# A recurrent block and two mixers on one core: early jobs placed anew, y of four chunks kept, table loaded first

## What is computed

```
cur      = (u * k_t) outer v_t
y_t      = r_t @ (state + cur)
state    = w_t[:, None] * state + k_t outer v_t
```

```
h   = gelu(x @ w_in)            # 384 -> 1024, tanh form
u,v = halves of h
v_n = (v - mean) / sqrt(var + 1e-6) * g_ln
v_s = w_sg @ v_n + b_sg         # over the 768 steps
x   = x + (u * v_s) @ w_out
```

## Time and profile before

| | us | share of the span |
|---|---|---|
| median of three runs | 441.37 | |
| the profiled execution | 443.14 | |
| its span, first to last instruction | 441.6 | |
| PE busy | 411.4 | 93% |
| DVE busy | 203.4 | 46% |
| POOL busy | 165.4 | 37% |
| ACT busy | 110.7 | 25% |
| mean granted clock of PE | 0.961 of full | |

### The profile page before, as it was taken

The page is one execution under the profiler, slowest core; times in us unless marked ns, Lnnn a source line. Parts: engine busy times, 40 slices in busy tenths (PEclk is TensorE's granted clock), DMA queues, the critical chain, the costliest instruction groups (busy, mean ns, idle before and its releaser), DMA issues.

```text
span 441.6 us, 6914 instructions
## 1 busy us (share of the span) xinstructions
PE 411.4 (93%) x2682; PEld 395.5 (90%) x2682; DVE 203.4 (46%) x414; ACT 110.7 (25%) x218; POOL 165.4 (37%) x174
## 2 busy tenths in 40 slices
PE   6869798878598999999999999999999999999997
PEld 5759788767497999998999999999999999999996
DVE  5747946766475595623165465635013113212311
ACT  3445222343524111205730021234013003201300
POOL 6746444635514484434769999200000000000000
PEclk9988958998888999999999999999999999999999
DMA  9997341505643100020021233000010000000000
GB/s 152 232 201 167 56 87 21 109 18 126 143 91 89 37 24 14 1 73 0 2 72 37 72 111 105 3 0 1 18 37 0 19 18 19 1 36 18 1 19 36
DMA packets 60130, 25.03 MB, mean 57 GB/s; under 512 B 51137, under 2 KB 58177, under 8 KB 60097
## 3 DMA queue, kind: packets, MB, share of 16 engines
q1 hardware_dynamic: 60096, 24.58, 24.6%
HBM read 22.22 MB, written 2.36 MB: 56 GB/s over the span
## 4 chain that ended last, share of the span: by engine, by line
PE 87%; DVE 6%; issue 3%; ACT 2%; POOL 0%; DVEq 0%; POOLq 0%; ACTq 0%
PE bank L1028 23%; PE bank L1030 23%; PE bank L1029 23%; PE bank L1118 4%; PE bank L1042 3%; PE bank L1079 3%; PE bank L1114 2%; PE bank L1151 2%; PE bank L1097 1%; PE bank L1086 1%; PE bank L1211 1%; DVE suf L808 1%; DVE pre L817 1%; PE bank L1169 1%; ACT vf L739 1%
## 5 line engine op out<-in xcount | busy, mean ns | idle before, releaser
L733 ACT ACTIVATE ha_hi<-bank 128x384 fp32r<-128x384 f32 x48 | 23.6, 492 | 113.1 <-PE bank L1030 113.1
L953 DVE SCALAR_TENSOR_TENSOR ha_lo<-bank,ha_hi 128x384 fp32r<-128x384 f32 x48 | 26.8, 557 | 50.2 <-ACT ha_hi L733 50.2
L1028 PE MATMUL bank<-c_hi,ha_lo 128*128 128x384 f32 x144 | 48.2, 335 | 0.0
L1030 PE MATMUL bank<-c_hi,ha_hi 128*128 128x384 f32 x144 | 48.1, 334 | 0.0
L1030 PE MATMUL bank<-u2T_hi,c_hi 128*128 128x384 f32 x144 | 48.1, 334 | 0.0
L1029 PE MATMUL bank<-c_lo,ha_hi 128*128 128x384 f32 x144 | 48.1, 334 | 0.0
L1028 PE MATMUL bank<-u2T_hi,c_lo 128*128 128x384 f32 x144 | 48.1, 334 | 0.0
L1029 PE MATMUL bank<-u2T_lo,c_hi 128*128 128x384 f32 x144 | 48.1, 334 | 0.0
L958 DVE TENSOR_TENSOR x<-bank,x 128x384 f32<-128x384 f32 x12 | 6.7, 557 | 65.3 <-PE bank L1030 65.3
L1028 PE MATMUL bank<-sg_hi,z_lo 128*128 128x384 f32 x96 | 32.7, 341 | 0.0
L1030 PE MATMUL bank<-sg_hi,z_hi 128*128 128x384 f32 x96 | 32.1, 334 | 0.0
(11 more groups left out here) (143 smaller groups left out, 932.8 us busy)
## 6 DMA issues: line engine op xcount, KB each, us to landing
raw<-in_moe_w_ch SPq DMA_DIRECT2D x12, 384.0 KB, 3.1
kc<-in_k SPq DMA_DIRECT2D x12, 192.0 KB, 4.3
rc<-in_r SPq DMA_DIRECT2D x12, 192.0 KB, 4.9
vn<-in_v SPq DMA_DIRECT2D x12, 192.0 KB, 4.4
raw<-in_moe_w_sg SPq DMA_DIRECT2D x6, 384.0 KB, 3.9
out<-x SPq DMA_DIRECT2D x12, 192.0 KB, 1.9
raw<-in_moe_w_in SPq DMA_DIRECT2D x4, 384.0 KB, 4.6
raw<-in_moe_w_tok SPq DMA_DIRECT2D x4, 384.0 KB, 3.1
```

The costliest lines, as they stand in the source:

```text
L733: sc.activation(ha[0][:, i, :], bank[:, 0:HALF], ACT.Relu).then_inc(act_out, 1)
L953: ve.scalar_tensor_tensor(ha[1][:, i, :], bank[:, 0:HALF], 0.0, ha[0][:, i, :].bitcast(F32), ALU.max, ALU.subtract).then_inc(dve_out, 1)
L1028: te.matmul(dst, left[1], right[0], start=first, stop=False)
L1030: return te.matmul(dst, left[0], right[0], start=False, stop=last)
```

## The change

Weight pieces w_in 2 and 3 are split one chunk later (chunks 2 and 3). YR becomes 4: y of four chunks waits for the test, the fourth in a part of `vf`; the count is made in chunk 3 ahead of the decays, two x tiles are written in chunk 3 and two in chunk 4. On POOL `diagonal_v(3)` and `diagonal_products(4)` stand ahead of the branch and `scale_r(4)` behind it, and `z_low` follows the splits. The shift of the normalisation is computed on POOL behind rstd. ACT loads the gelu table by a one-column activation before anything else and does `normal` before the jobs of slot 1. DVE does slot 1 before the state and `stats` behind the next diagonal. The table of slots is written anew: v and u a little later, each `wsg` with a `u` between it and the next, two `sg` jobs in the tail instead of the chunks.

```diff
--- before.py
+++ after.py
@@ -33,7 +33,7 @@
 PIECE = 768
 SLOTS = 3
 WR, KR, VR = 2, 2, 3
-YR = 3
+YR = 4
 BANKS = 8
 PJ = S // PART
 RAW = H * PJ * D
@@ -58,18 +58,17 @@
 
 
 SLOT = {
-    (4, 0): [("xT", 0, 0), ("xT", 0, 1)], (4, 1): [("xT", 0, 2), ("v", 0, 0)], (4, 2): [("u", 0, 0)],
-    (5, 0): [("xT", 0, 3), ("v", 0, 1)], (5, 1): [("v", 0, 2)], (5, 2): [("xT", 0, 4), ("u", 0, 2)],
-    (6, 0): [("v", 0, 3)], (6, 1): [("v", 0, 4), ("u", 0, 4)], (6, 2): [("xT", 0, 5), ("wsg", 0, 0), ("wsg", 0, 1)],
-    (7, 0): [("v", 0, 5)], (7, 1): [("u", 0, 6), ("wsg", 0, 2), ("wsg", 0, 3)],
-    (7, 2): [("wsg", 0, 4), ("wsg", 0, 5), ("wsg", 0, 6), ("wsg", 0, 7)],
-    (8, 0): [("u", 0, 1)], (8, 1): [("u", 0, 3), ("wsg", 0, 8), ("wsg", 0, 9)],
-    (8, 2): [("u", 0, 5), ("wsg", 0, 10), ("wsg", 0, 11)],
-    (9, 0): [("u", 0, 7)], (9, 1): [("sg", 0, 0)], (9, 2): [("sg", 0, 1)],
-    (10, 0): [("sg", 0, 2)], (10, 1): [("sg", 0, 3)], (10, 2): [("sg", 0, 4)],
-    (11, 0): [("sg", 0, 5)], (11, 1): [("sg", 0, 6)],
+    (4, 0): [("xT", 0, 0), ("xT", 0, 1)], (4, 2): [("v", 0, 0)],
+    (5, 0): [("v", 0, 1), ("xT", 0, 2)], (5, 1): [("xT", 0, 3)], (5, 2): [("u", 0, 0)],
+    (6, 0): [("v", 0, 2), ("xT", 0, 4)], (6, 1): [("v", 0, 3), ("wsg", 0, 0)], (6, 2): [("u", 0, 2), ("wsg", 0, 1)],
+    (7, 0): [("v", 0, 4), ("xT", 0, 5)], (7, 1): [("wsg", 0, 2), ("u", 0, 4), ("wsg", 0, 3)],
+    (7, 2): [("u", 0, 6), ("wsg", 0, 4)],
+    (8, 0): [("v", 0, 5)], (8, 1): [("wsg", 0, 5), ("u", 0, 1), ("wsg", 0, 6)], (8, 2): [("u", 0, 3), ("wsg", 0, 7)],
+    (9, 0): [("wsg", 0, 8), ("u", 0, 5)], (9, 1): [("wsg", 0, 9), ("u", 0, 7)], (9, 2): [("wsg", 0, 10), ("wsg", 0, 11)],
+    (10, 0): [("sg", 0, 0)], (10, 1): [("sg", 0, 1)], (10, 2): [("sg", 0, 2)],
+    (11, 0): [("sg", 0, 3)], (11, 1): [("sg", 0, 4)],
 }
-TAIL = ([("sg", 0, 7)] + [("xT", 1, i) for i in range(6)] + [("out", 0, i) for i in range(6)]
+TAIL = ([("sg", 0, i) for i in range(5, 8)] + [("xT", 1, i) for i in range(6)] + [("out", 0, i) for i in range(6)]
         + [("v", 1, i) for i in range(6)] + [("u", 1, i) for i in range(8)] + [("sg", 1, i) for i in range(8)]
         + [("tok1", 0, i) for i in range(2)] + [("out", 1, i) for i in range(6)] + [("tok2", 0, i) for i in range(6)]
         + [("tok1", 1, i) for i in range(2)] + [("uT", 0, i) for i in range(6)] + [("tok2", 1, i) for i in range(6)]
@@ -90,7 +89,7 @@
     for n, job in enumerate(ORDER):
         a += "A" in OUT_BY[job[0]]
         d += "D" in OUT_BY[job[0]]
-        bank = 6 + n % 2 if n < EARLY else (n - EARLY) % BANKS
+        bank = 6 + n % 2 if n < EARLY else (n - EARLY + 6 + EARLY % 2) % BANKS
         at[job] = (n, a, d, bank)
     return at
 
@@ -174,7 +173,7 @@
     sbd = put("sbd", [PART, 2, NP, 2 * D])
     st = put("st", [PART, NP, D])
     rku = put("rku", [PART, H, D])
-    yt = put("yt", [PART, YR, C])
+    yt = put("yt", [PART, YR - 1, C])
     ub = put("ub", [PART, C])
     cmask = put("cmask", [PART, PART])
     ones = put("ones", [PART, PART])
@@ -233,6 +232,7 @@
             sem("suf_done"), sem("inverted"), sem("pre_done"), sem("kp_done"), sem("masked"), sem("su_done"),
             sem("st_done"), sem("dg_done"), sem("y_done"), sem("x_out"))
         kn_copied, rt_copied, sbd_done, checked = sem("kn_copied"), sem("rt_copied"), sem("sbd_done"), sem("checked")
+        table_in = sem("table_in")
         rp_done, rk_done, rku_done, base_done, flagged = (sem("rp_done"), sem("rk_done"), sem("rku_done"),
                                                           sem("base_done"), sem("flagged"))
         ok_marked, ok_summed, ok_total, ok_counted = (sem("ok_marked"), sem("ok_summed"), sem("ok_total"),
@@ -321,6 +321,9 @@
 
         def v_jobs(n):
             return [(b, i) for s in range(SLOTS) for kind, b, i in slot_jobs(n, s) if kind == "v"]
+
+        def y_place(n):
+            return vf[:, 2, 0:C] if n == YR - 1 else yt[:, n % (YR - 1), :]
 
         def vf_tile(b, tc):
             return vf0[:, tc - 3, :] if b == 0 and tc >= 3 else vf[:, tc % 3, :]
@@ -550,8 +553,8 @@
                 wait_ring(pool, v_in, n)
                 pool.wait_ge(dg_done, n + 1)
                 if n >= YR:
-                    pool.wait_ge(x_out, n - YR + 1)
-                gp.tensor_tensor(yt[:, n % YR, :].rearrange("p (h d) -> p h d", h=H),
+                    pool.wait_ge(x_out, n - YR + 2)
+                gp.tensor_tensor(y_place(n).rearrange("p (h d) -> p h d", h=H),
                                  vn[:, n % VR, :].rearrange("p (h d) -> p h d", h=H),
                                  dg[:, :].rearrange("p (h a) -> p h a", a=1).to_broadcast([PART, H, D]), ALU.mult
                                  ).then_inc(base_done, 1)
@@ -562,6 +565,9 @@
                 gp.tensor_scalar(rstd[:, tc:tc + 1], mv[:, tc, 1:2], 1e-6, None, ALU.add).then_inc(rstd_a, 1)
                 pool.wait_ge(rstd_a, n + 1)
                 gp.tensor_tensor(rstd[:, tc:tc + 1], rstd[:, tc:tc + 1], nhalf[:, :], ALU.pow).then_inc(rstd_done, 1)
+                pool.wait_ge(rstd_done, n + 1)
+                gp.tensor_scalar(shift[:, tc:tc + 1], mv[:, tc, 0:1], rstd[:, tc:tc + 1], -1.0, ALU.mult, ALU.mult
+                                 ).then_inc(shifted, 1)
 
             def z_low(b, tc):
                 n = NC * b + tc
@@ -583,7 +589,7 @@
                 gp.tensor_tensor(gt[1][:, dt, at_], src, gt[0][:, dt, at_].bitcast(F32), ALU.subtract
                                  ).then_inc(g_split, 1)
 
-            early = {1: ("w_in", 2), 2: ("w_in", 3), 4: ("w_in", 0), 5: ("w_in", 1), 9: ("w_out", 0), 10: ("w_out", 1)}
+            early = {2: ("w_in", 2), 3: ("w_in", 3), 4: ("w_in", 0), 5: ("w_in", 1), 9: ("w_out", 0), 10: ("w_out", 1)}
 
             def chunk(n):
 
@@ -592,14 +598,17 @@
                     rstd_tile(b, i)
                 if n + 1 < NCH:
                     diagonal_products(n + 1)
-                for b, i in v_jobs(n - 2):
-                    z_low(b, i)
+
+            def chunk_end(n):
+
                 if n in early:
                     split_high(*early[n])
                 if n + 1 < NCH:
                     scale_r(n + 1)
                 if n in early:
                     split_low(*early[n])
+                for b, i in v_jobs(n - 1):
+                    z_low(b, i)
                 for s in range(SLOTS):
                     for kind, b, i in slot_jobs(n, s):
                         if kind == "sg":
@@ -608,10 +617,12 @@
             def rest():
 
                 gp.tensor_copy(flag[:, :], nhalf[:, :]).then_inc(flagged, 1)
-                diagonal_v(YR)
-                for n in range(YR + 1, NCH):
+                chunk_end(YR - 1)
+                for n in range(YR, NCH):
                     chunk(n)
-                split_gated(0, 7)
+                    chunk_end(n)
+                for i in range(5, 8):
+                    split_gated(0, i)
                 split_piece("tok1", 0)
                 split_piece("tok1", 1)
                 for tc in range(NC):
@@ -632,10 +643,10 @@
 
             scale_r(0)
             diagonal_products(0)
-            for n in range(YR):
+            for n in range(YR - 1):
                 chunk(n)
-            diagonal_products(YR + 1)
-            scale_r(YR + 1)
+                chunk_end(n)
+            chunk(YR - 1)
             pool.wait_ge(ok_counted, 1)
             pool.wait_ge(preset, 3)
             n_ok = pool.value_load(oki[0:1, 0:1])
@@ -675,9 +686,7 @@
 
             def check_range(i):
 
-                if i == 0:
-                    act.wait_ge(v_consts, V_CONSTS)
-                else:
+                if i:
                     act.wait_ge(checked, CHECK_ORDER.index(i))
                 if i < NC:
                     c = 2 * (i // 2)
@@ -710,6 +719,8 @@
                     n = NC * b + i
                     if b:
                         act.wait_ge(z_split, n - 2 if i >= 3 else i + 1)
+                    elif i == 2:
+                        act.wait_ge(x_out, YR)
                     sc.activation(vf_tile(b, i), bank[:, :], ACT.Gelu_apprx_tanh).then_inc(act_out, 1)
                 elif kind == "u":
                     ft, th = i // 2, i % 2
@@ -755,6 +766,9 @@
                     wait_dve_out(act, "out", 0, tc)
                 sc.copy(x1[0][:, tc, :], x[:, b, tc, :]).then_inc(x1_hi, 1)
 
+            act.wait_ge(v_consts, V_CONSTS)
+            sc.activation(junk[:, 0:1], w_low[:, :], ACT.Gelu_apprx_tanh).then_inc(table_in, 1)
+            act.wait_ge(table_in, 1)
             take_r(0)
             check_range(0)
             check_range(1)
@@ -767,12 +781,12 @@
                     take_r(n + 1)
                 for i in checks.get(n, ()):
                     check_range(i)
+                for b, i in v_jobs(n - 1):
+                    normal(b, i)
                 for job in slot_jobs(n, 1):
                     take_job(*job)
                 if n % NC < NC - 1:
                     take_state(n)
```

(55 more changed lines are left out.)

## The result

The changed kernel ran in 410.38 us (median of four runs, 410.02 to 413.81), the kernel before in 442.23 (four runs, 438.6 to 445.87): a ratio of 0.932 with a 95% interval of 0.924 to 0.941. The forecast was 416, with 405 to 432 around it. The profiled executions took 443.14 and 410.41 us, a difference of 32.7 where the sum said 26.6. Runs of one kernel differ with the mean clock that PE was granted in them: the changed kernel took 410.02 us at 1.00 and 413.81 at 0.987.

What follows compares the result with a forecast made beforehand. PE bounds the kernel: full after 182.8 us, before that 37 us lost to idle time and low clock. Terms 7.2 + 0 + 22.4 - 3 = 26.6 us off the profiled 443.14 gave 416.5, stated as 416, range 405 to 432.

Steps and rivals of the forecast that it cites:

- Step 1: w_in 2 split in chunk 2: the 4.1 us gap before its scores and 3.1 of low clock go; 7.2 us.
- Step 2: Test and x tiles of chunk 3: POOL blocks an x tile, PE's 2.2 us gap for the state stays; 0.
- Rival A: x tiles get through or wait for one POOL instruction; PE's gap under 1 us; 409 us; chance 0.15.
- the term of the clock behind the gap: Behind chunk 3's wait for the state: of 6.5 us lost to low clock, 5.2 stay lost, 1.3 are freed.
- The undisturbed end of the state, +3.5: Chunk 3: without a disturbance the state ends 3.5 us after the start of rp(4), against +5.8 before.
- Step 3: Slots, normalisation and shift: PE's waits for xT, shift and wsg evictions go, with their clock losses; 22.4 us, 3 kept back.
- Step 4: Shift on POOL: 3.6 us of POOL work, in the tail or in chunks where POOL idles; 0.
- Step 5: Gelu table first: a load of 1.28 us moves to the start, from where ACT waited for PE anyway; 0.
- Step 6: Two sg jobs to the tail, about 3.1 us each, from one stretch with PE full to another; 0.
- Rivals B: wsg evictions still late in chunks 5 to 9, 15 us come back: 431 to 432 us; chance 0.20.
- C: DVE and POOL cost a gap of 2 us or more in each chunk: about 436 us; chance 0.08.
- D: SP's queue starves the chunks of k, r and v behind raw pieces: 455 us; chance 0.05.

Runs made afterwards that it cites:

- the test at its old place: Changed kernel with the test of the decays, its three x tiles, count and branch in chunk 3 as before (YR = 3): 411.26 us.
- the weight piece alone: Kernel before with only w_in 2 split in chunk 2 and w_in 3 in chunk 3 behind the diagonal term: 433.72 us against 439.10.
- the control: The changed kernel unaltered, run as the yardstick of the experiments: 410.02 us.
- the tiles freed: Changed kernel with POOL's low split in chunks 3 and 4 waiting until that chunk's two x tiles are written: 406.75 us.

## Why the prediction was right, and where its sizes were off

**Step 1, the weight piece**, 7.2: the scores moved by 6.7 in the trace; 5 to 6 by the runs. Right.

**Step 2, the x tiles.** The mechanism came as written: a blocked x tile, the state late (5.1 us behind the start of rp, for 5.8 before and 5.7 forecast), PE's gap of 1.75 where 2.2 was kept. That POOL is the cause is shown twice, by taking the split away and by delaying it. Rival A is thereby refuted as a mechanism, though the time came out nearer its 409 than the 416. The step that failed is the term of the clock behind the gap: 5.2 us left lost, because the kernel before ran 10 us at 1.2 GHz there. The changed kernel's profile has 3.4 us at 1.2 GHz, 1.65 us by the same count, and the traces put its cost at nothing, since DVE paces chunk 4. The term took the low clock for a fixed consequence of the gap, and it is not: behind the same wait of 2.19 us the profile of the kernel before and that of the test at its old place show some 10 us at 1.2 GHz and that of the weight piece alone none; behind 1.75 us the changed kernel's shows 3.4 us and the control's none. What decides it, no run here shows. The two x tiles moved into chunk 4 were costed at 0, or 1.3 at worst; freeing them there was worth 1.6 us of the 3.3, and on DVE's time. The undisturbed end of the state, +3.5, is 3.7 by the terms written beside it; with the tiles freed it was +3.35, and nothing in the sum hangs on it.

**Step 3, slots, normalisation, shift**, 22.4 less 3 kept back. The waits named are gone, and from chunk 6 on PE's busy time was the bound, as the comparison of 12.3 with 10.8 us a chunk said. The 3 us kept back for overlooked gaps were too much: from the scores of chunk 2 to the last sg job PE is idle for 3.05 us, 1.75 of it step 2's gap, so 1.3 in all the rest, 0.36 of that before an sg job. The margins of the wsg pairs held; each of the three parts undone brings waits back.

**Step 4**, the shift on POOL: no cost seen; PE shows no wait for it. **Step 5**, the table, 0: wrong, it is 1.3 at full clock. I took the cover from the kernel before, where ACT waited for PE; in the new order the gelu of v0 has the statistics and the mask behind it. **Step 6**: 0, right; the last part lasts 255.5 us as before, and no load was late.

Where the missing 6.1 us are can be counted in the two traces. The prediction left 10.4 us of idle time and clock in the chunks (2.2, 5.2 and 3); the changed kernel has 4.7 (3.05 idle, 1.65 clock). Of these 5.7 us, 3.5 are the clock, 0.5 the gap and 1.7 the reserve. Rivals B, C and D show nothing in the trace: no wsg wait, no wait for DMA.

The time lies at the lower edge of the forecast's own 410 to 424, and some of the distance is the execution that was profiled. The sum started from 443.14 us, an execution with 10 us of low clock in chunk 4; other executions of the kernel before, at a mean clock of 0.969 and 0.973, took 437.1 and 437.3. Against those the change saves about 27 us, against the median 32. No trace of such a fast execution exists, so which stretch of low clock it lacked is an inference.

## What to carry to other kernels

When a chain of small waits bounds a stretch, cost each wait by what it is waiting for. Then count each engine's busy time per round: where PE was the busiest by 1.5 us a chunk, nearly all of the waits could go; in the one chunk where DVE was busy 12.60 of 12.70 us, neither a full clock nor a filled gap on PE gave anything, and only DVE's time counted. Do not carry the low clock of one profile over to the new kernel as if it belonged to the gap before it; look at several executions. An instruction of one column can hold DVE for 2.68 us when it starts in the middle of a POOL product and a second POOL instruction is ready behind it; put a wait on the one that nobody needs. And a cover must be looked up in the new order, not in the old.

## What the runs showed of the hardware

A DVE instruction with two SBUF inputs that starts in the middle of a POOL product waited for that product alone when POOL's next instruction was not ready (two x tiles in 1.49 us), and for the next one too when it was (3.26 us; a shift of one column 2.68 us in two kernels). The Trainium skill, "SBUF — State Buffer", section "Who interferes with whom", has the lock held for one instruction by whoever issued first; the traces agree with that for the lone product and go beyond it for the pair.

The clock differs from run to run of one kernel: 410.0 us at 1.0, 410.4 at 0.995, 413.8 at 0.987, the same program. Behind the same wait of 2.19 us PE ran 10 us at 1.2 GHz in one profile and at full clock in another. The kernel with the x tiles freed, where PE's list has no wait for the state, had 1.0 in each of its four runs, and 0.4 us between them; the control, with a wait of 1.75, had 1.0 in three of four, so that the freed tiles keep the clock up is not shown by this.
